# Attention and two feed-forward layers on one core: a new order of the opening, with five weight halves moved from GpSimd to VectorE

## The reference, cut to what matters

```
k_p = k.reshape(B, H, Sp, 8, D).mean(axis=3)         # B 8, H 8, S 576, Sp 72, D 64
v_p = v.reshape(B, H, Sp, 8, D).mean(axis=3)
attn = softmax(q @ k_p.T / sqrt(D));  x = attn @ v_p   # x becomes 4608 tokens x 512
h = x @ w_in1                                         # 512 x 2048
g = where(h >= 1, h, where(h <= -1, 0, (h + 1)**2 / 4))
y = g @ w_out1                                        # 2048 x 512
out = (relu(y @ w_in2)**2) @ w_out2
```

## Time and profile before

| | |
|---|---|
| median of 3 runs | 1609.3 us (1608.44 to 1610.39) |
| the profiled execution's own time | 1610.46 us |
| its span in the trace | 1608.7 us |
| PE busy in the span | 1575.4 us, 98% |
| DVE, ACT, POOL busy | 1134.0, 834.1, 253.8 us |

### The profile page before, as it was taken

One profiled execution on the slowest core, in us unless ns is written; L12 is line 12 of the kernel. 1 busy time (PEld: TensorE's weight loads), 2 busy tenths in 40 slices (PEclk: granted clock), 3 DMA queues, 4 the chain that ended last, 5 costly groups with the idle time before them and its releaser, 6 DMA issues.

```text
span 1608.7 us, 25303 instructions
## 1 busy us (share of the span) xinstructions
PE 1575.4 (98%) x9216; PEld 1557.7 (97%) x9216; DVE 1134.0 (70%) x1758; ACT 834.1 (52%) x1443; POOL 253.8 (16%) x358
## 2 busy tenths in 40 slices
PE   5799999999999999999999999999999999999999
PEld 4699999899999999999999999999999999999999
DVE  6566657766665778678778876676667987876874
ACT  3566666766656754444434764344446653443442
POOL 6716516934530000000000000000000000000000
PEclk9899999999999999999999999999999999999999
DMA  7246658746644843442452724433447744245241
GB/s 243 101 161 232 208 178 280 257 167 230 230 163 130 257 138 119 157 143 94 157 168 86 283 104 145 145 126 139 147 144 250 242 157 151 90 153 185 75 135 40
DMA packets 174460, 265.92 MB, mean 165 GB/s; under 512 B 15616, under 2 KB 152832, under 8 KB 174336
## 3 DMA queue, kind: packets, MB, share of 16 engines
q1 hardware_dynamic: 174336, 264.30, 49.1%
HBM read 157.29 MB, written 106.95 MB: 164 GB/s over the span
## 4 chain that ended last, share of the span: by engine, by line
PE 93%; DVE 3%; POOL 1%; ACT 1%; issue 1%; DMA 1%; SPq 0%; DVEq 0%; POOLq 0%; ACTq 0%
PE bank L769 41%; PE bank L667 24%; PE bank L792 22%; PE bank L634 2%; PE bank L644 1%; PE bank L645 1%; DVE gf L1165 1%; DVE b L1158 1%; DVE prob L1114 1%; PE bank L659 0%; PE bank L657 0%; PE bank L658 0%; PE bank L656 0%; DMA k_raw<-k 0%; POOL wi_lo L548 0%
## 5 line engine op out<-in xcount | busy, mean ns | idle before, releaser
L769 PE MATMUL bank<-gf,f_hi 128*128 128x384 f32 x2688 | 682.1, 334 | 0.4 <-DVE u_b L1175 0.3
L769 PEld LDWEIGHTS bank<-gf,f_hi 128*128 128x128 f32 x2688 | 484.6, 188 | 1.2 <-DVE u_b L1175 0.7
L769 PE MATMUL bank<-gf,f_lo 128*128 128x384 f32 x1344 | 448.9, 334 | 0.0
L892 ACT ACTIVATE gf<-b 128x768 fp32r<-128x768 f32 x336 | 278.6, 845 | 265.2 <-PE bank L769 177.0
L1165 DVE TENSOR_TENSOR gf<-b,gf 128x768 fp32r<-128x768 f32 x336 | 314.4, 951 | 43.3 <-ACT gf L892 43.3
L792 PE MATMUL bank<-xf,w_hi 128*128 128x384 f32 x1344 | 341.0, 334 | 0.0
L667 PE MATMUL bank<-x_hi,wi_hi 128*128 128x384 f32 x768 | 268.2, 349 | 4.3 <-DVE x_lo L1126 4.3
L667 PE MATMUL bank<-x_lo,wi_hi 128*128 128x384 f32 x768 | 259.5, 338 | 0.0
L667 PE MATMUL bank<-x_hi,wi_lo 128*128 128x384 f32 x768 | 259.3, 338 | 0.0
L769 PEld LDWEIGHTS bank<-gf,f_lo 128*128 128x128 f32 x1344 | 252.3, 188 | 0.0
L792 PEld LDWEIGHTS bank<-xf,w_hi 128*128 128x128 f32 x1344 | 242.8, 188 | 0.0
(11 more groups left out here) (90 smaller groups left out, 1495.4 us busy)
## 6 DMA issues: line engine op xcount, KB each, us to landing
b<-g_dram SPq DMA_DIRECT2D x192, 384.0 KB, 4.1
g_dram<-g_st SPq DMA_DIRECT2D x192, 192.0 KB, 2.0
g_dram<-c_st SPq DMA_DIRECT2D x192, 192.0 KB, 1.9
s_dram<-su_s SPq DMA_DIRECT2D x24, 512.0 KB, 2.9
k_raw<-k SPq DMA_DIRECT2D x32, 288.0 KB, 3.5
q_sb<-q SPq DMA_DIRECT2D x48, 192.0 KB, 2.7
y_dram<-o_st SPq DMA_DIRECT2D x48, 192.0 KB, 1.9
x_raw<-y_dram SPq DMA_DIRECT2D x24, 384.0 KB, 4.7
```

What stands on the lines that cost most here:

```text
L769: last = mm(dst[:, 0:H], w[:, 2 * i + kt, cols], x[:, half, kt, :], start=q_ < 3 and i == 0 and kt == 0 and h == 0, stop=q_ >= 4 and i == ...
L892: copy(gf[layer][r % GRING][:, 0], unit_source(n)[:, 2 * i:2 * i + 2, :], ACT.Copy).then_inc(gf_hi, 1)
```

## The change

It changes only the order of the lists in the opening (chunk 0 and the pairs of chunk 1), who makes five of the low halves, and one small instruction of ACT.

- POOL: in the opening the averages and low halves of values come first. Low halves `wi_lo` 0 to 4 leave the list, and 5 to 15 stand behind `values_low(4)`, between the blocks 5 to 7 and behind them.
- DVE: makes `wi_lo` 0 to 4, behind `tokens_low` of pair 0 (tile 0), 1 (tiles 1 and 2), 2 (tile 3) and 3 (tile 4). `normal(0)` stands ahead of `keys(2)`, and `below(a + 2)` and `normal(a + 1)` are written around `probabilities_low(a)`: the sum and the product of the next pair come ahead of `pT_lo`, and the scores of pair 4 are taken up in the opening. `normal(4)` stands behind `wi_lo` 4.
- PE: scores run three pairs ahead; `first_hidden(0)` moves behind `scores(4)`; `values(3)`, `first_hidden(2)` and `first_hidden(3)` follow each other. The pairs 4 to 7 have their step 0 in slots 0, 3, 6, 9 where they had it in -4, 0, 4, 8; from pair 8 on nothing changes. Pair 4's steps 0 to 2 are in the opening, its transposes now follow `hidden(3)` and its values `hidden(5)`. In a slot the hidden product now stands first, then values, transposes, scores.
- ACT: an exponential of one column first of all. `weights_high(1)` to `(6)` stand behind `values_high` and ahead of `tokens_high` of the same turn.
- SP: key blocks and weight tiles are loaded earlier in the list relative to the value blocks 2 to 5, whose loads wait for POOL.

```
@@ POOL
-            weights_low(0)
-            values(1)
...
-            for g in range(-4, SLOTS):
+            for m in range(1, 5):
+                if m < 4:
+                    spread_keys(m + 1)
+                values(m)
+                values_low(m)
+            for m, more in ((5, (5, 6)), (6, (7, 8)), (7, (11, 12))):
+                spread_keys(m)
+                for j in more:
+                    weights_low(j)
+                values(m)
+                for j in {6: (9, 10), 7: (13,)}.get(m, ()):
+                    weights_low(j)
+                values_low(m)
+            weights_low(14)
+            weights_low(15)
+            for g in range(SLOTS):
                 slot(g)
@@ PE
+            def first_weights(j):
+                if j < WI_FIRST:
+                    pe.wait_ge(wi_ready_first, j + 1)
+                else:
+                    pe.wait_ge(wi_ready, j - WI_FIRST + 1)
...
+                for a in pairs_at(g, 5):
+                    values(a)
+                for a in pairs_at(g, 3):
+                    transposes(a)
+                for a in pairs_at(g, 0):
                     scores(a)
@@ ACT
+            act.wait_ge(mask_made, 1)
+            copy(warm[:, :], half_sb[:, :], ACT.Exp)
@@ DVE
+            def weights_low(j):
+                dve.wait_ge(wi_hi_ready, j + 1)
+                vec.tensor_tensor(wi_lo[j][:, :], wi_raw[j][:, :], wi_hi[j][:, :].bitcast(F32), ALU.subtract)\
+                    .then_inc(wi_ready_first, 1)
...
+                tokens_low(a)
+                for j in ((0,), (1, 2), (3,), (4,))[a]:
+                    weights_low(j)
+            normal(4)
@@ shared
+        def pairs_at(g, step):
+            first = {4: 0, 5: 3, 6: 6, 7: 9}
+            return [a for a in range(HP, PAIRS) if first.get(a, 4 * (a - 5)) + step == g
+                    and (a > HP or step > 2)]
```

More of the change, by code:

```diff
@@ L686, in first_hidden @@
                     if kt == 0:
-                        pe.wait_ge(wi_ready, g + 1)
+                        first_weights(g)
                     hidden_part(g, kt)
             def slot(g):
[L691 to L694, removed]
+                hidden(g)
+                for a in pairs_at(g, 5):
[3 more added lines that the diff above has]
+                for a in pairs_at(g, 0):
                     scores(a)
[L696 to L699, removed]
             pe.wait_ge(ident_made, 2)
@@ L706, in _ @@
             values(0)
[L707 to L715, removed]
+            transposes(1)
+            scores(3)
+            values(1)
+            transposes(2)
+            scores(4)
+            first_hidden(0)
+            values(2)
+            transposes(3)
+            first_hidden(1)
+            values(3)
+            first_hidden(2)
+            first_hidden(3)
+            for g in range(HRING, SLOTS):
                 slot(g)
@@ L928, in slot @@
             def slot(g):
[L929 to L933, removed]
+                for a in pairs_at(g, 4):
+                    probabilities(a)
+                for a in pairs_at(g, 6):
+                    tokens_high(a)
                 for m in keys_in(g - 4):
-                    if m > 5:
+                    if m > 7:
                         values_high(m)
@@ L947, in slot @@
                     copy(g_st[g % GST][:, :], g_st[g % GST][:, :], ACT.Square).then_inc(act_ready, 1)
-                if t == 1 and is_later(a):
+                for a in pairs_at(g, 1):
                     exps(a)
@@ L1231, in slot @@
             def slot(g):
-                a, t = pair_in(g), g % 4
-                if t == 0 and is_later(a - 1):
-                    probabilities_low(a - 1)
-                if t == 1 and is_later(a):
+                for a in pairs_at(g, 4):
+                    probabilities_low(a)
+                for a in pairs_at(g, 1):
                     below(a)
-                if t == 2 and is_later(a - 1):
-                    tokens_low(a - 1)
-                if t == 2 and is_later(a):
+                for a in pairs_at(g, 6):
+                    tokens_low(a)
+                for a in pairs_at(g, 2):
                     normal(a)
@@ L1275, in _ @@
             below(0)
+            normal(0)
+            below(1)
             keys(2)
-            normal(0)
             for a in range(HP):
                 if a + 1 < HP:
-                    below(a + 1)
+                    normal(a + 1)
                 probabilities_low(a)
-                if a + 1 < HP:
-                    normal(a + 1)
-                tokens_low(a)
+                if a + 2 <= HP:
+                    below(a + 2)
                 if a + 3 < 6:
                     keys(a + 3)
+                tokens_low(a)
+                for j in ((0,), (1, 2), (3,), (4,))[a]:
+                    weights_low(j)
+            normal(4)
             for g in range(-4, SLOTS):
```

76 lines of the change are left out of this document (27 added, 49 removed).

## The result

The changed kernel takes 1595.9 us (median of four executions, 1594.51 to 1598.54), the kernel before, measured beside it, 1609.4 (1608.44 to 1610.39). The ratio is 0.9918, 95% interval 0.9901 to 0.9935: 13.5 us faster. Predicted were 1596.0 us and a gain of 13.3. The profiled execution took 1594.51 us (span 1592.7), 1.4 under the median, where that of before was 1.2 over its own.

What follows compares the result with a forecast made beforehand. The prediction took POOL's list as the chain holding PE back up to hidden(4), with PE the bound behind it. hidden(4) 14.8 us earlier, less 1.5 owed, gave 13.3: 1609.3 - 13.3 = 1596.0 us, range 1591.5 to 1601.5.

Steps and rivals of the forecast that it cites:

- step 3: From x_lo to hidden(3): DVE's list takes 5.3 us (bounds 4.0 and 6.5), so hidden(3) starts at 42.7, 16.0 earlier.
- Step 1: POOL up to v_bd of block 4: 43.88 - 11.2 + 1.0 + 1.2 = 34.9 us, 9.0 earlier.
- At its worst: Blocking between POOL and DVE's five moved halves: 2.1 us less gain, 1.6 of POOL's time and 0.5 of DVE's.
- Step 2: From v_bd of block 4 to first_hidden(3): 1.5 + 1.6 us, so PE starts it at 38.0 and x_lo starts at 37.4.
- Step 4: From hidden(3) to hidden(4): 6.3 us, lower clock for hidden(3) and transposes; hidden(4) starts at 49.0, 14.8 earlier.
- Step 5: PE behind hidden(4): pair 4's values, 0.9 us, and pair 5's transposes, 0.6, still owed; 14.8 - 1.5 = 13.3 us.
- main case: Whole kernel: gain of 13.3 us, 1596.0 us, with its own range of 1594 to 1599; chance 0.68.
- rival 2: Opening: the clock stays up and the collisions are few, gain 17 us, 1592.3 us; chance 0.14.
- signs of being wrong: Block 2's v_raw waiting over 2 us for DMA, DVE's wi_lo over 1.5 each, PE waits in slots 5 to 16 or later.
- What was costed at nothing: Pairs' spacing, tiles 5 to 15 made by POOL, pair 7's tokens, the early exponential and SP's stores: no cost.
- Rival 1: Opening: DVE becomes the bound at 7.8 us a turn, gain 5.4 us, 1603.9 us; chance 0.11.
- Rivals 3 and 4: 3: POOL and ACT hand-over in slots, 1615 us, chance 0.03; 4: gain waited for again, within 0.2% of 1609, 0.04.

Runs made afterwards that it cites:

- repeated run: The changed kernel run again with no edit, against the kernel before: 1595.6 us, ratio 0.9912.
- filler kernel: The changed kernel with twelve matmuls more on PE behind first_hidden(3), 2.24 us, result not used: 1596.45 us, ratio 0.9912 against the kernel before.

## Why the prediction was right

**The bound.** PE waits in the opening, and POOL's list is the chain up to `v_bd` of block 4: both were right. That it is the chain all the way to `hidden(4)` was not: halves and POOL's list alone, in the old order of the rest, bring that `v_bd` 5.0 us forward and give 4.5 us of 14. Behind it DVE's list sets `hidden(3)`, which step 3 of the prediction did have.

**Step 1** gave 34.9 for `v_bd` of block 4; it was 35.89 and, repeated, 35.14. The sum held better than its terms. From the first `v_bd` on the stretch is 25.28 us where it was 32.25, 7.0 less, and I had 9.0. By term, from POOL's rows: six halves and a spread out, 7.9 as predicted. The waits for `v_hi` fell by 1.8 (2.84 to 1.00), where I took 2.3. The wait for key sums was to fall by 1.0 and rose by 1.2 (0.45 + 0.60 + 1.13 against 1.02), because DVE does a pair's sum and product and a weight half ahead of them: this is the term that was wrong in that execution. The load of value block 2 cost 0 and not 1.0. POOL's turns with DVE, summed as what its instructions take over their shortest, are 2.0 us where they were 0.5: 1.5 against the 1.2 of the sum. The last 1.0 us comes from ahead of the stretch, where the first `v_bd` ends at 10.61 and not 11.62; in the repeated run it ends at 11.69, so that part is the luck of an execution. There the stretch is 23.45 us, 8.8 less: the wait for `v_hi` is 0.53, as the prediction left it, the only wait for key sums 0.60, and the turns are 2.3. So of the terms the turns were too small in both profiles (1.5 and 1.8 more than before, for 1.2), the waits were off in one, and that 34.9 fits both sums is in part luck.

The Trainium skill's rule in "SBUF — State Buffer", "Who interferes with whom", says that a VectorE instruction with two SBUF inputs and a GpSimd one that reads SBUF shut each other out for a whole instruction. The runs agree: 0.68 against 1.78 us for one shape above. At its worst it was to cost 2.1 us more than the sum had, and it cost less: 0.3 and 0.6 us more of turns in step 1, and 0.1 in step 3. The same section of the Trainium skill says that a `tensor_scalar` can be shut out too, under conditions, and a `tensor_reduce` on this chip can't. The runs agree: `total` of six columns took 0.17 us at 21.93 and 0.63 at 40.27 in the first profile of the change, and 1.32 at 292.26 in the filler kernel's, while the reductions keep their 0.59 beside a busy POOL.

**Step 2** gave 0.6 us from `x_lo` to PE and 2.5 from `v_bd` to `x_lo`; measured 38.33 - 35.89 = 2.4. PE had no wait there at all: `first_hidden(3)` ran straight behind `first_hidden(2)`.

**Step 3** gave 5.3 us from `x_lo` to `hidden(3)`; it took 5.4. `hidden(3)` started at 43.74, 42.98 when repeated, for 42.7.

**Step 4** gave 6.3 us with the lower clock for part of it. With the lower clock it took 5.40, with the upper 3.86 (3.8 were given for that). I had the lower level last through the transposes, and it ended 0.3 us ahead of them.

**Step 5** gave 1.5 us owed; PE's busy time behind the mark rose by 1.54.

In the repeated run the sum is 63.81 - 48.38 - 1.5 = 13.9 for 13.3 predicted, and its profiled time is 13.6 under that of before. In the first profile it is 16.2 - 1.5 = 14.7, and 1.8 more come from waits for `prob` at 100 to 800 us that this execution happened not to have (0.5 for 2.3), less 0.5 us of other rows, which I can't place: 15.95. So the main case describes the median, and the profiled execution lies between it and rival 2: it has that rival's clock, and not its few collisions. Of the signs of being wrong one came in part: the first `wi_lo` of DVE took 1.66 us (at 19.72), the next two 2.68 together, the last two 0.75 and 0.92.

**What was costed at nothing.** The loads: right. The early exponential: up to 1.2 us at `hidden(4)`, hidden in the spread of executions. Tiles 5 to 15 ahead of their slots: right in the changed kernel, where they stand between the blocks, and the run with eight of them in one row shows the price without that cover, 3.02 us and an idle ACT. The pairs' spacing was not tried by itself.

**The rivals.** Rival 1 (DVE becomes the bound) was close: POOL already waits 2.2 us for DVE's key sums in the first profile (0.6 in the repeated run), and five halves more cost 7 us. Rival 2's clock came in one profile of two, its few collisions in none. Rivals 3 and 4 did not come: PE waits for no `wi_lo` or `x_lo` in the slots 5 to 16.

The gain in parts, as far as the runs carry it (the parts need not add up, since they were taken in different orders): 4.5 us from the halves and POOL's list in the old order; 4.1 (2.9 between the profiles) from putting pair 4's transposes and values behind `hidden(3)`, taken out of the final order; 5 to 6, or a little more, are left for the rest of DVE's, ACT's and PE's order and the spacing, which were not run one by one; which of them carries it is open. In the new order the halves alone carry 3.1.

## What to carry to other kernels

Find the chain that sets when the busiest engine gets going, but then ask for each thing on that engine what it waits for and whether it has to stand there: POOL's new list, with the five halves on DVE, gave 4.5 us with the other lists as they were and 14 with the new ones. Work that is taken off a chain must be put where nothing waits behind it; with eight such instructions in one row 6 of 7.7 us were lost again. When an instruction goes to another engine, count what the new engine's own consumers wait for (the sums of keys here), not only its busy time.

## What the runs showed of the hardware

- One VectorE subtraction of 128x512 from two SBUF operands takes 0.68 us where nothing holds it up and as much as 1.78 beside GpSimd, whose 1.29 became 1.84 beside it; a six-column `tensor_scalar` goes from 0.17 to 1.32. Reductions and instructions that read a bank (0.55 us) stay as they are.
- Such turns part executions of this kernel as much as the clock does. The two profiles of the changed kernel differ by 2.4 us: 1.7 are PE's waits for `prob` between 100 and 800 us (0.5 and 2.2), 1.5 the lower clock behind `hidden(3)`, and 0.8 go the other way, by an earlier `hidden(3)`.
- The same idle 2.8 us of PE was followed by the lower clock level for 3.4 us in one execution and not in the other. With PE kept busy there for 2.2 us, the mean clock was 0.999 or more in all four executions; that the filler is the cause is not shown. An idle 2.51 us in another kernel was followed by the lower level too.
- The granted clock reads 1.00 from the start, though matmuls over 384 columns start 0.32 us apart up to 25 us in the first profile, the distance that they have at 0.50, and 0.17 from 29.3 us on.
- The table load of ScalarE takes 1.28 us wherever it stands (it starts at 0.74 us with the early exponential, at 8.09 without it).
